# An order change at the seam between plain and Winograd products in a fused attention and expert kernel

## The reference

```python
def _moe_ref(x, domain_probs, w1, w2):
    p = domain_probs / (domain_probs.sum(-1, keepdims=True) + 1e-09)
    out = np.zeros((N, D), dtype=np.float32)
    for e in range(E):
        h = np.maximum(x @ w1[e], 0.0)
        out += p[:, e:e + 1] * (h @ w2[e])
    return out.astype(np.float32)

def reference(...):
    attn_out = _attn_ref(**attn_kwargs)          # 2 x 8 heads x 576 x 64
    x = attn_out.transpose(0, 2, 1, 3).reshape(B * S, H * D)   # 1152 x 512
    x = _moe_ref(x=x, **moe_kwargs)              # w1: 4 x 512 x 1024, w2: 4 x 1024 x 512
    return _moe2_ref(x=x, **moe2_kwargs)         # h = x @ w_in; g = P(h) / Q(h); g @ w_out
```

## Time and profile before

| | us |
|---|---|
| median of 3 runs | 638.96 (636.57 to 639.53) |
| the profiled execution, whole | 636.57 |
| its span, first to last instruction | 634.8 |
| PE busy | 629.0 |
| DVE / ACT / POOL busy | 399.1 / 324.4 / 292.0 |

### The profile page before, as it was taken

How to read it: one execution, slowest core, us unless ns; L and a number is a source line. 1 busy time by engine, 2 the same in 40 slices (tenths; PEclk the granted TensorE clock), 3 DMA queues, 4 the chain that set the end, 5 groups by cost and what they waited for, 6 DMA issues and landing times.

```text
span 634.8 us, 10710 instructions
## 1 busy us (share of the span) xinstructions
PE 629.0 (99%) x3986; PEld 558.6 (88%) x3986; DVE 399.1 (63%) x774; ACT 324.4 (51%) x752; POOL 292.0 (46%) x307
## 2 busy tenths in 40 slices
PE   8999999999999999999999999999999999999997
PEld 7888889888898888898988998889899899988996
DVE  6546884547655356235356235448988788889896
ACT  6887743344212343112343112346887777777774
POOL 5786647882112783202783101154622675732221
PEclk9999999999999999999999999999999999999999
DMA  9964202222100222100222100111610000001011
GB/s 271 295 166 150 86 34 69 97 67 68 35 0 4 85 80 66 35 1 8 80 79 67 33 2 7 62 47 53 232 69 0 2 0 2 1 0 51 2 50 50
DMA packets 22771, 39.76 MB, mean 63 GB/s; under 512 B 3584, under 2 KB 4224, under 8 KB 22720
## 3 DMA queue, kind: packets, MB, share of 16 engines
q1 hardware_dynamic: 22720, 39.09, 19.4%
HBM read 36.72 MB, written 2.36 MB: 62 GB/s over the span
## 4 chain that ended last, share of the span: by engine, by line
PE 96%; ACT 2%; DVE 1%; POOL 0%; issue 0%
PE banks L813 47%; PE banks L785 25%; PE banks L726 19%; PE banks L698 2%; ACT scratch L948 1%; PE banks L679 1%; PE banks L669 1%; PE banks L849 1%; PE banks L686 1%; ACT scratch L958 0%; DVE acc L1320 0%; POOL scratch L1638 0%; ACT x_hi L962 0%; PE banks L821 0%; DVE scratch L1244 0%
## 5 line engine op out<-in xcount | busy, mean ns | idle before, releaser
L813 PE MATMUL banks<-w_hi,h 128*128 128x512 f32 x512 | 169.8, 395 | 0.0
L1415 DVE TENSOR_TENSOR stage<-banks,stage 128x320 f32<-128x320 f32 (+1 forms) x140 | 64.1, 461 | 91.0 <-PE banks L785 86.8
L813 PEld LDWEIGHTS banks<-w_hi,h 128*128 128x128 f32 x512 | 96.2, 188 | 20.6
L813 PE MATMUL banks<-w_lo,h 128*128 128x512 f32 x256 | 101.2, 395 | 0.0
L1698 POOL TENSOR_TENSOR w_lo<-raw,w_hi 128x512 fp32r<-128x512 f32 x32 | 41.4, 1316 | 128.5 <-ACT w_hi L1004 128.5
L1712 POOL TENSOR_TENSOR h_lo<-rational,h_hi 128x384 fp32r<-128x384 f32 x47 | 47.6, 1013 | 108.7 <-ACT h_hi L1206 108.7
L726 PE MATMUL banks<-x_hi,w_hi 128*128 128x384 f32 (+1 forms) x256 | 84.9, 331 | 0.0
L1049 ACT ACTIVATE h<-stage 128x320 fp32r<-128x320 f32 (+1 forms) x84 | 37.0, 447 | 92.3 <-DVE stage L1415 91.9
L726 PE MATMUL banks<-x_lo,w_hi 128*128 128x384 f32 (+1 forms) x256 | 82.7, 323 | 0.0
L726 PE MATMUL banks<-x_hi,w_lo 128*128 128x384 f32 (+1 forms) x256 | 82.5, 322 | 0.0
L1422 DVE SCALAR_TENSOR_TENSOR h<-stage,h 128x320 fp32r<-128x320 f32 (+1 forms) x84 | 58.2, 705 | 25.7 <-ACT h L1049 24.1
(11 more groups left out here) (143 smaller groups left out, 1493.9 us busy)
## 6 DMA issues: line engine op xcount, KB each, us to landing
raw<-in_weights SPq DMA_DIRECT2D x48, 256.0 KB, 2.9
raw<-in_weights SPq DMA_DIRECT2D x20, 512.0 KB, 3.6
raw_last<-in_weights SPq DMA_DIRECT2D x16, 256.0 KB, 5.9
scratch<-in_v SPq DMA_DIRECT2D x16, 192.0 KB, 6.1
scratch<-in_qk_dil SPq DMA_DIRECT2D x8, 320.0 KB, 5.5
out_t<-acc SPq DMA_DIRECT2D x9, 256.0 KB, 2.1
scratch<-in_qk_plain SPq DMA_DIRECT2D x8, 272.0 KB, 5.2
scratch<-in_qk_rest SPq DMA_DIRECT2D x2, 256.0 KB, 4.9
```

The source lines that it names most:

```text
L813: last = nc.tensor.matmul(sum_bank(k, t), h[:, cols], w[:, f, :], start=f == 0 and i == 0, stop=f == FC - 1 and i == 2)
L1415: nc.vector.tensor_tensor(out, bank, to, ALU.add).then_inc(combined, 1)
```

## The change

Three engines get a new order around the first Winograd pairs; no instruction is added, taken away or altered.

- PE: in pair (KW, 0) tile 0 of the outer product of chunk 7 of iteration 1 goes from behind S3 T3 to behind A12 B21, and tile 1 from behind S4 B22 to behind S3 T3.
- ACT: in pair (KW, 0) `high_pair(0, 2)` goes from behind C11 to ahead of T4's high part; `high_pair(0, 3)` from behind the snapshot of pair (KW, 1) to behind C22 of pair (KW, 0); `high_pair(1, 0)` from the end of pair (KW, 1) to behind its C22; `high_pair(1, 1)` and `(1, 2)` from behind C22 to ahead of C22 in pairs (KW, 2) and (KW, 3).
- DVE: `take_sum(KW - 1, 0)` goes from behind the combination C22 to ahead of U2, `take_sum(KW - 1, 1)` from the end of the pair to the place behind the combination C22.

```diff
@@ PE
             winograd_product(KW, 0, "A11 B11")
             outer_of_pair(KW, 0, 0)
-            for name in FIRST_PRODUCTS[1:5]:
+            winograd_product(KW, 0, "A12 B21")
+            outer_product(KW - 1, FC - 1, range(0, 1))
+            for name in FIRST_PRODUCTS[2:5]:
                 winograd_product(KW, 0, name)
-            outer_product(KW - 1, FC - 1, range(0, 1))
+            outer_product(KW - 1, FC - 1, range(1, 2))
             for name in FIRST_PRODUCTS[5:]:
                 winograd_product(KW, 0, name)
-            outer_product(KW - 1, FC - 1, range(1, 2))
@@ ACT
                     snapshot(k, p)
-                    if (k, p) == (KW, 0):
+                    if k == KW and p == 0:
+                        high_pair(0, 2)
                         high_t(0, 1, "T4")
-                    if (k, p) == (KW, 1):
-                        high_pair(0, FP - 1)
                     high_quarter(k, p, "C11")
-                    if (k, p) == (KW, 0):
-                        high_pair(0, 2)
                     high_t_of_step(t_step(k, p, 0))
                     if is_first(k) and p == 0:
                         high_pair(e, FP - 1)
-                    if is_last(k) and p and k > KW:
+                    if is_last(k) and p and (k, p) != (KW, 1):
                         high_pair(e + 1, p - 1)
                     high_quarter(k, p, "C22")
-                    if k == KW and p > 1:
-                        high_pair(1, p - 1)
+                    if (k, p) == (KW, 0):
+                        high_pair(0, FP - 1)
+                    if (k, p) == (KW, 1):
+                        high_pair(1, 0)
...
                     high_quarter(k, p, "C21")
                     high_quarter(k, p, "C12")
-                    if (k, p) == (KW, 1):
-                        high_pair(1, 0)
@@ DVE
             low_t(0, 1, "T4")
+            take_sum(KW - 1, 0)
             for k in range(KW, START[MOE]):
...
                     combine(k, p, "C22")
                     if (k, p) == (KW, 0):
-                        take_sum(KW - 1, 0)
+                        take_sum(KW - 1, 1)
                     low_quarter(k, p, "C22")
...
-                    if (k, p) == (KW, 0):
-                        take_sum(KW - 1, 1)
```

## The result

| | before | after |
|---|---|---|
| median of 20 executions each, us | 637.33 (636.16 to 639.73) | 640.75 (639.23 to 643.52) |
| ratio, 95% interval | | 1.0051 (1.0038 to 1.0064) |
| the profiled execution, us | 636.57 | 639.12 |
| its span, us | 634.8 | 637.2 |
| from the first Winograd matmul to the end, us | 549.62 | 552.26 |

The change costs 3.4 us in the medians and 2.55 us between the two profiled executions (2.4 in the spans). The last row of the table leaves out the attention stage, whose length varies from execution to execution by itself, so it compares the edited part alone: 2.64 us.

The account below looks back on a forecast made before the run. PE was taken to bound the kernel. Waits of 2.1 less 0.04 plus 0.4 us gave +2.5: 639.1 us from the profiled 636.57, or 641.4 from the median 638.96; range 637.3 to 643.8.

Parts of the forecast that it names:

- What bounds the kernel: Whole run: PE busy 629.0 of 634.8 us; a better order in the edited stretch could give back under 0.2 us.
- The collision on T4: First pair: POOL's early low parts of weight pair 2 stretch DVE's making of T4, so S3 T3 waits 2.1 us.
- +2.8: Total delay in us if DVE and POOL lock each other out for whole instructions, making T4 about 0.3 us later.
- Pair 3: Weight pair 3's early POOL instruction stretches C21's low part on DVE; A12 B21 of pair 1 starts 0.4 us later.
- rival 2: Pair 3's raw weights reload late, holding up ACT, the snapshot and PE: +4.3 us, median 643.3; chance 0.08.
- The sum, +2.5: Whole change: 2.1 us at S3 T3, less 0.04, plus 0.4 at A12 B21 of pair 1.
- rival 4: TensorE's granted clock falls in the 2 us pause, adding to the forecast; no price given, chance 0.05.
- The predicted time, 641.4: Forecast median in us: 638.96, the median of three executions, with the +2.5 us delay added.
- within: Outcome that the measured time lies inside 0.5%, 3.2 us, of no change; chance 0.69.
- slower: Outcome that the kernel is measured slower by more than 0.5%, 3.2 us; chance 0.29.
- signs for wrong: New profile: L1372 at 0.49 us, S3 T3 at 90.8, over 1 us at pair 1, shifts under 1 or over 3.2, clock under 1.00.
- more room: Expert 1's weight pairs: POOL 2.4 us earlier and PE 2.5 us later, so no further wait was expected there.

Follow-up runs that it names:

- e8: Kernel before, with both tiles of the outer product of chunk 7 between S3 T3 and A22 T4; 637.72 against 637.32 us, ratio 1.0006.
- e3: Changed kernel with ACT's order as before, only PE's and DVE's lists changed; 636.82 against 637.57 us, ratio 0.9988.
- e7: e5's kernel with POOL's last instruction for weight pair 2 making one of three low parts; one execution, 640.39 us.
- e4: Kernel before with ACT's part of the change alone; 640.68 us, ratio 1.0054.
- e9b: Changed kernel with POOL's second low part of weight pair 2 waiting until T4's low part is made; 641.26 us, ratio 1.0062.
- e1: Changed kernel again, unaltered, for a second set of executions; 640.12 against 637.57 us, ratio 1.0046.
- e10b: e9b's kernel with weight pair 3 also back behind the snapshot of pair (KW, 1) on ACT; 638.62 against 637.31 us, ratio 1.0017.
- e5: Changed kernel with weight pair 3 back behind the snapshot of pair (KW, 1) on ACT; one execution, 642.83 us (before: 637.32).
- e6: Changed kernel with weight pair 2 back behind C11 on ACT, pair 3 left at its new place; one execution, 644.59 us.
- e2: Changed kernel with nine 128x128 identity matmuls ahead of S3 T3, filling PE's pause; 640.74 us, ratio 1.0052.
- e11: e10b's kernel with high_pair(1, 0) also back behind C12 of pair (KW, 1); 637.53 against 637.83 us, ratio 0.9996.

## Where the prediction was right, and where not

**What bounds the kernel, and what there was to gain: right.** I gave the better order under 0.2 us. e8 took the long step at A22 T4 away and e3 the one at S3 T3, a later step grew in both, and neither was faster than before by more than its interval (ratios 1.0006 and 0.9988).

**The collision on T4: right, mechanism and size.** I put T4's end at 90.62; it is 90.41, and the whole of PE is 0.21 us earlier in that profile (first Winograd matmul 84.95 against 85.16). U2 92.22, now 92.02. S3 T3 2.1 late, now 2.08. The rule "ends 0.35 after the POOL instruction that runs when it starts" held at each place: 0.34 and 0.35 here, 0.35 in e7. e4 and e3 show that ACT's move alone makes it, e7 that it goes with the length of POOL's instruction.

I had weighed the rule of the Trainium skill, page SBUF — State Buffer, section "SBUF: two separate sides", by which the port pair is an exclusive lock for the whole instruction, the first to start keeping the other out, and had read it as +2.8. The profile agrees on the length of the blocking (2.03 us in place of 0.49), and by the recorded starts also on the order: L1334 had started at 87.31, ahead of L1701 at 87.96, and ended at 88.34, and L1701 took 0.26 longer than its 1.84; L1370 started at 88.38, behind L1701, and waited for its end. So what was wrong was my reading, that L1701 would keep out an instruction which had been waiting since before it. The measured 2.62 lies between +2.5 and +2.8 and by itself wouldn't have told them apart; the row of L1334 does.

**Pair 3: right in mechanism, the term mis-sized by a little.** C21's low part lies in POOL's L1701, and A12 B21 is 0.54 late (predicted 0.4, started 99.23 for 99.4). The reload took what I had taken (freed at 88.00, data used 3.66 later at 91.66; I had 3.63), so rival 2 is out. My sentence that this delay would be 2.1 if the first were absent is borne out by e9b: 2.2, with 0.55 of the first left.

**The sum, +2.5: right for the profile** (2.55 and 2.64); **what is missing in it is the clock.** That is rival 4. I named the clock in the pause, found no row that priced it, and left it at a chance of 0.05 with no price. In 20 of 30 executions it came, and when it comes it costs 0.8 us net: 1.4 us lost to slow matmuls less the second pause, which they swallow. 20/30 of 0.8 is 0.5 us. The medians of the first set lie 3.4 apart, 0.9 over the sum, and 0.4 of that stays without a cause; those of e1's set lie only 2.55 apart. The mean span of all 30 executions of the changed kernel is 2.75 us over that of the 59 of the kernel before that have one on record. So a further cause is not shown, and none is needed. The rule to draw: the rows showed a pause of 1.1 us without loss, and I took that as if it spoke for 2.1. It said nothing about it.

**The predicted time, 641.4, is near the measured 640.75 by two errors that offset each other.** I took the median of three executions, 638.96, as the base. Over 20 it is 637.33, 1.6 lower. The effect was taken 0.9 smaller than these medians have it. That the two nearly cancel is luck. The error of the base is the larger one: with three values of 636.57, 638.96 and 639.53 in hand, their spread (0.46%) was as large as the effect. The change is +0.51% with an interval from 0.38% to 0.64%: it sits on the bound of 0.5% that I had named, so "within" with 0.69 was no better grounded than "slower"; with rival 4 priced I should have split them evenly.

**What the new profile would show:** all signs came (L1370 at 88.38 with 2.03 us, T4's high part at 90.44, U2 at 92.02, the long step of PE, the C21 row, the smaller gap at pair 1, and the old pace behind it). Of the signs for wrong, one came in part: a clock under 1.00, in other executions than the profiled one.

**The late collision of e10b: not foreseen.** I had passed over `high_pair(1, 0)` with "more room". In the changed kernel that is true, since the two pauses give it that room; once they are gone it is the third of the same kind, 1.5 us in e10b.

## What to carry to other kernels

When an instruction is moved to where its engine idles, ask what its successor on a *third* engine will then run beside: here ACT's move cost ACT nothing, and woke POOL just where DVE was making an operand in SBUF that PE needs; in this kernel a DVE instruction with two inputs in SBUF that starts inside a POOL one lasts until POOL is done and a third of a microsecond more. Price a new stop of TensorE not by the stop alone: behind the stops of about 2 us here the clock often fell too, so look at the mean clock of all executions and not only at the profiled one. And before a change of half a per cent is forecast from a median of three, see how far the three lie apart.

## What the runs showed of the hardware beside that

- **TensorE's clock fell behind stops of about 2 us, in some executions only.** With the stop of 1.98 us (2.08 with the step behind it) it was lower in 20 of 30 executions of the changed kernel and in all five of e4, with the 2.1 us of e9b in five of six, and in the one of e5; with e6's 4.45 us in its one. Of the 47 executions of e2, e3, e7, e8, e10b and e11, whose stops in the profiles are 1.23 us or less or filled by matmuls, one was at 0.998 and none lower, and of the kernel before none was under 0.999. Where in the execution it fell only the profiled ones show: the stretch at 1.2 GHz lasts 3.4 us in e1, e4, e5 and e9b and begins 0.5 (e5) to 1.05 us (e4) after the restart; in e6 it lasts 6.8 us and begins 1.0 us before the restart. What decides in which execution it comes no run showed.
- **POOL's instruction pays as well, when DVE's is under way first.** It takes 0.93 to 1.05 us in place of 0.74 (L1687 of the changed kernel and of e1), and 2.10 in place of 1.84 (L1701 of 87.96). The L1701 of 96.45, which DVE's C21 met only after its start, took its 1.84 all the same, and so did e9b's (1.82). An instruction of DVE with one input in PSUM isn't touched.
- **The spread between executions comes from the first 20 us.** The first Winograd matmul stands at 84.95 to 85.16, at about 85.8 or at 87.5 to 87.6 us in the profiled executions, and the spans of the kernel before come in groups around 634.8, 635.7 and 637.5, which lie apart by about as much as these starts. In the late form the first matmuls of the attention stage run at the slow pace. The same 16 matmuls, in e2 (late form):

```profile
8.63 0.92 PE L669 MATMUL banks<-scratch 64*64 64x96 f32 x16
```

and in the kernel before (early form):

```profile
7.79 0.56 PE L669 MATMUL banks<-scratch 64*64 64x96 f32 x16
```

The mean granted clock doesn't show this: it reads 1.000 for e2 too. Comparing tails, from one named matmul to the end, takes this spread out; the medians above still hold it.
